# Routed experts on TensorE: 28 steps of two 64-row pieces on two column halves, in place of 31 steps of one 128-row tile

## The reference, cut to what matters

```python
def _moe2_ref(x, w_gate, w_local, w1, w2):
    logits = np.einsum('bsd,de->bse', x, w_gate)
    local_gate = 1.0 / (1.0 + np.exp(-np.einsum('bsd,de->bse', x, w_local).squeeze(-1)))
    for b in range(B):
        prev_e = -1
        for s in range(S):
            fresh_e = int(np.argmax(logits[b, s]))
            if s == 0 or local_gate[b, s] < 0.5:
                e = fresh_e
            else:
                e = prev_e if prev_e >= 0 else fresh_e
            prev_e = e
            ...
            h = np.maximum(x[b, s] @ w1[e], 0.0)
            out[b, s] = p[e] * (h @ w2[e])
```

## Time and profile before

| What | Value |
|---|---|
| Median of 3 runs | 992.57 us (991.91 to 993.82) |
| The profiled execution: its own time | 993.9 us |
| Its span | 992.2 us |
| Granted clock of PE, mean over the span | 0.987 of 2.4 GHz |
| PE busy with matmuls | 947.2 us, 95% of the span |
| DVE, ACT, POOL busy | 465.9, 270.5, 275.8 us |

### The profile page before, as it was taken

The page is one execution under the profiler, slowest core; times in us unless marked ns, Lnnn a source line. Parts: engine busy times, 40 slices in busy tenths (PEclk is TensorE's granted clock), DMA queues, the critical chain, the costliest instruction groups (busy, mean ns, idle before and its releaser), DMA issues.

```text
span 992.2 us, 51897 instructions
## 1 busy us (share of the span) xinstructions
PE 947.2 (95%) x23581; PEld 732.5 (74%) x23582; DVE 465.9 (47%) x964; ACT 270.5 (27%) x503; POOL 275.8 (28%) x297
## 2 busy tenths in 40 slices
PE   4689999999999999999999999999999999999995
PEld 3579989899898996454554554557888888888884
DVE  5447877887887762423143143162352322222220
ACT  1224444444444442201202202202212122122120
POOL 4535566556656651000011010010052101111111
PEclk9789999999999999999999999999999999999999
DMA  5216442333333321780100100047421111001000
GB/s 147 64 50 209 140 123 89 114 104 119 96 115 111 89 72 41 238 271 0 38 27 24 42 28 20 1 133 256 130 88 61 34 34 39 23 28 33 27 29 3
DMA packets 57704, 81.63 MB, mean 82 GB/s; under 512 B 22274, under 2 KB 37454, under 8 KB 57648
## 3 DMA queue, kind: packets, MB, share of 16 engines
q1 hardware_dynamic: 33536, 58.87, 19.0%
q10 hardware_dynamic: 21088, 13.32, 5.2%
q0 software_dynamic: 3024, 8.72, 2.4%
HBM read 68.04 MB, written 14.45 MB: 83 GB/s over the span
## 4 chain that ended last, share of the span: by engine, by line
PE 91%; issue 3%; DVE 2%; DMA 2%; POOL 1%; ACTq 0%; ACT 0%; POOLq 0%; SPq 0%; DVEq 0%
PE ps_D L1478 14%; PE ps_D L224 12%; PE ps_G L1460 6%; PE ps_E L1460 6%; PE ps_B L236 5%; PE ps_E L956 5%; PE ps_B L188 3%; PE ps_G L1467 3%; PE ps_D L1039 3%; PE ps_A L930 3%; PE ps_G L188 3%; PE ps_D L990 2%; PE ps_E L954 2%; PE ps_E L188 2%; PE ps_D L930 2%
## 5 line engine op out<-in xcount | busy, mean ns | idle before, releaser
L1478 PE MATMUL ps_D<-room,hT 128*128 x496 | 139.1, 433 | 0.8 <-issue 0.8
L224 PE MATMUL ps_D<-room 128*128 128x384 f32 x384 | 126.7, 489 | 0.6 <-DVE room L291 0.6
L1478 PEld LDWEIGHTS ps_D<-room,hT 128*128 128x128 f32 x496 | 91.8, 190 | 35.9 <-issue 1.3
L224 PEld LDWEIGHTS ps_D<-room 128*128 128x128 f32 x384 | 72.1, 190 | 51.5 <-issue 1.6
L1421 POOL DMA_INDIRECT out<-y,token x31 | 35.6, 1147 | 258.3 <-DVE y L1585 224.7
L550 POOL DMA_INDIRECT sorted_rows<-rows,slot x24 | 23.9, 997 | 278.3 <-DVE slot L542 272.2
L894 POOL TENSOR_TENSOR room<-room 32x256 f32<-32x256 f32 x96 | 69.5, 724 | 106.5 <-DVE room L1310 101.1
L1521 ACT ACTIVATE hT<-ps_G 128x512 f32<-128x512 f32 x31 | 18.5, 598 | 217.6 <-PE ps_E L1467 211.4
L1585 DVE TENSOR_SCALAR y<-ps_D,x_in 128x320 f32<-128x320 f32 x31 | 17.0, 550 | 125.9 <-PE ps_D L1478 117.5
L1568 DVE COPY w_own<-room 128x1024 f32 x62 | 44.9, 729 | 62.3 <-PE ps_G L1460 33.8
L291 DVE TENSOR_TENSOR room<-ps_D,room 128x384 f32<-128x384 f32 x32 | 17.8, 558 | 113.2 <-PE ps_D L224 107.8
(11 more groups left out here) (225 smaller groups left out, 1646.2 us busy)
## 6 DMA issues: line engine op xcount, KB each, us to landing
room<-in_moe_w SPq DMA_DIRECT2D x8, 1280.0 KB, 12.6
room<-in_moe_w SPq DMA_DIRECT2D x8, 1024.0 KB, 9.2
room<-in_kb SPq DMA_DIRECT2D x48, 160.0 KB
room<-in_vt SPq DMA_DIRECT2D x24, 320.0 KB, 3.1
x_in<-sorted_rows ACTq DMA_DIRECT2D x27, 161.0 KB, 2.3
room<-in_w SPq DMA_DIRECT2D x48, 82.7 KB
room<-in_a SPq DMA_DIRECT2D x48, 80.0 KB
room<-in_r SPq DMA_DIRECT2D x48, 80.0 KB
```

Of the source, the lines that this page charges most:

```text
L224: mm = pe.matmul(self.vs_bank[n % 2][:, 0:TH], self.v[:, s, d * P:(d + 1) * P], self.wspT[:, s, t * TH:(t + 1) * TH], start=(s == 0), stop ...
L1478: mm = pe.matmul(self.ps_y, side.hT[:, u % 2, f, :], self.weights.w2[:, bass.ds(e, 1), f, :], start=(f == 0), stop=(f == self.NF - 1))
```

## The change

A piece is now 64 rows, so that at most 48 + 7 = 55 pieces are needed, and a step takes two pieces, which may belong to different experts: 28 steps (`STEPS`). The two pieces share a step's buffers: rows 0 to 63 and 64 to 127 of `x_in`, of `ps_y` and of the output.

- `hidden`: four quarters instead of two halves: the two pieces times the two halves of the inner features. Each matmul has 64 weight columns and 64 moving columns, and consecutive matmuls alternate between the column halves of the array (outputs at partitions 0 and 64). `w1_own` stays one buffer, so DVE copies each half twice a step (`fetch_w1` with its piece `h`). `w1_rest_own` gets a place for each piece, and the 64-feature part is done for both pieces together behind the four quarters, on four 64x64 tiles.
- `project`: the first piece reads w2 of its expert out of `room`, on the first column half; the second piece reads `w2_own`, a copy that ACT makes once a step (`fetch_w2`), on the second. PE reads its register before `hidden`.
- `fetch`: two table reads and two DMAs of 64 rows.
- The waits of `hidden` and `project` are gathered on a semaphore instruction of its own (`passed`) ahead of the matmuls.
- The tables hold 56 pieces; the first part covers 24 (12 steps) instead of 11 tiles. The operations of the tables have more elements.
- The routing steps of the fourth batch stand at other places (`steps` in `tensor`, `scalar`, `vector`), most of them inside a step, ahead of `project` on PE. `other_tiles` is split in two (`blank_rows` and `other_tiles`), and POOL scatters after 6 puts instead of 3.
- The scratch area for POOL's DMA descriptors is set to 4096 bytes, which makes room for `w2_own`.

```diff
+STEPS = (SORTED_HALVES + 1) // 2
...
-FIRST = (BATCH - 1) * TILES - (EXPERTS - 1)
-NT = 32
+FIRST = 12
+NT = 2 * STEPS
...
     def fetch(self, eng, turn, u):
+        for h in range(2):
+            at = eng.value_load(self.side.tile_at[0:1, bass.ds((turn * self.SLOTS + u) * 2 + h, 1)], min_val=0,
+                                max_val=BLANK_HALF)
+            eng.dma_start(self.side.x_in[h * HALF:(h + 1) * HALF, u, :],
+                          self.by_half[bass.ds(at, 1), :, :].rearrange("o p n -> (o p) n")).then_inc(self.s_in[u], 16)
...
     def hidden(self, pe, turn, u):
...
+        for h in range(2):
+            tokens = slice(h * HALF, (h + 1) * HALF)
+            x = side.xTt[:, u % 2, :, tokens]
+            for half in range(2):
+                pe.wait_ge(self.w1_in, 4 * t + 2 * h + half + 1)
+                if h == 0:
+                    pe.wait_ge(self.h_out, self.FREE + 2 * t + half - 1)
+                pe.sem_inc(self.passed, 1)
+                for f in range(4):
+                    for k in range(NK - 1):
+                        for c in range(2):
+                            lo = (half * 4 + f) * P + c * HALF
+                            mm = pe.matmul(self.ps_h[half][c * HALF:(c + 1) * HALF, f, tokens],
+                                           side.w1_own[:, k, lo:lo + HALF], x[:, k, :],
+                                           start=(h == 0 and f == 0 and k == 0), stop=False, skip_group_check=True)
+                mm.then_inc(self.h_made, 1)
+        pe.wait_ge(self.w1_rest_in, 2 * t + 2)
+        pe.sem_inc(self.passed, 1)
+        for h in range(2):
+            tokens = slice(h * HALF, (h + 1) * HALF)
             for f in range(4):
+                for half in range(2):
+                    kept = slice(half * self.REST, (half + 1) * self.REST)
+                    for c in range(2):
+                        lo = f * P + c * HALF
+                        mm = pe.matmul(self.ps_h[half][c * HALF:(c + 1) * HALF, f, tokens],
+                                       side.w1_rest_own[kept, h, lo:lo + HALF], side.xTt[kept, u % 2, NK - 1, tokens],
+                                       start=False, stop=True, skip_group_check=True)
...
+    def project(self, pe, turn, u, e):
...
+        pe.wait_ge(self.w2_in, t + 1)
...
         for f in range(self.NF):
+            pe.matmul(self.ps_y[first, :], side.hT[:, u % 2, f, first], self.weights.w2[:, bass.ds(e, 1), f, :],
+                      start=(f == 0), stop=(f == self.NF - 1))
+            mm = pe.matmul(self.ps_y[second, :], side.hT[:, u % 2, f, second], side.w2_own[:, f, :],
                            start=(f == 0), stop=(f == self.NF - 1))
...
+    def fetch_w2(self, act, turn, u):
+
+        side, w2, t = self.side, self.weights, turn * self.SLOTS + u
+        e = act.value_load(side.tile_expert[0:1, bass.ds(2 * t + 1, 1)], min_val=0, max_val=self.E - 1)
+        w2.until_loaded(act, e)
+        if not isinstance(turn, int) or t >= 1:
+            act.wait_ge(self.y_made, t)
+        act.activation(side.w2_own[:, :, :], w2.w2[:, bass.ds(e, 1), :, :].rearrange("p o f n -> p (o f) n"),
+                       ACT.Copy).then_inc(self.w2_in, 1)
...
+    def fetch_w1(self, dve, turn, u, h):
...
+            if h == 1:
+                dve.wait_ge(self.h_made, self.part_made(t, 0, half))
+            elif later:
+                dve.wait_ge(self.h_made, self.part_made(t - 1, 1, half))
...
+        steps = {1: routing.turn_rows, 4: routing.turn_back, 5: routing.count}
...
+        steps = {1: turned_rows, 3: lambda: routing.join_rows(act, self.LAST),
+                 4: lambda: routing.copy_expert(act, self.LAST), 5: lambda: routing.copy_counts(act, self.LAST)}
...
+        steps = {0: lambda: routing.choose(dve, self.LAST), 2: lambda: routing.scan(dve, self.LAST),
+                 4: lambda: routing.weigh(dve, self.LAST), 5: lambda: routing.place(dve, self.LAST),
+                 6: lambda: routing.blank_rows(dve), 7: lambda: routing.other_tiles(dve)}
```

More of the change, by code:

```diff
@@ L39 @@
 FIRST_END = 25088
[L40 to L43 removed]
+CAP = TOKENS // HALF
+BLANK_HALF = EXPERTS * CAP
+FIRST = 12
+NT = 2 * STEPS
 PAY = DM + 2
@@ L555, in later @@
         sb = Carver(c.wide, 0, 2 * SEQ)
-        return (sb("over", EXPERTS, CAP), sb("past", NT, EXPERTS), sb("weighed", NT, EXPERTS), sb("te", NT),
-                sb("at", NT), sb("count", EXPERTS), sb("tiles", EXPERTS), sb("upto", EXPERTS), sb("weight", EXPERTS),
+        later = NT - 2 * FIRST
+        return (sb("over", EXPERTS, CAP), sb("past", later, EXPERTS), sb("weighed", later, EXPERTS), sb("te", later),
+                sb("at", later), sb("count", EXPERTS), sb("tiles", EXPERTS), sb("upto", EXPERTS), sb("weight", EXPERTS),
                 sb("need", EXPERTS), sb("blank", PAY))
@@ L627, in other_tiles @@
         dve.tensor_copy(s.blank_slot[:, :], need[:, :]).then_inc(self.blank_slot_d, 1)
+    def other_tiles(self, dve):
+        s, c, link = self.side, self.made, self.link
+        over, past, weighed, te, at, count, tiles, upto, weight, need, blank = self.later(c)
         link(dve, dve.tensor_tensor(weight[:, :], s.first[:, 1:EXPERTS + 1], tiles[:, :], ALU.subtract))
@@ L632, in other_tiles, with fill_blank_half @@
         link(dve, dve.tensor_tensor_scan(upto[:, :], s.ones[:, 0:EXPERTS], tiles[:, :], 0.0, ALU.mult, ALU.add))
-        self.table(dve, c, upto[:, :], weight[:, :], FIRST, SORTED_TILES - FIRST, s.first[:, 0:1], self.all_known)
-    def fill_blank_tile(self, sp):
+        self.table(dve, c, upto[:, :], weight[:, :], 2 * FIRST, NT - 2 * FIRST, s.first[:, 0:1], self.all_known)
+    def fill_blank_half(self, sp):
         blank = self.later(self.made)[-1]
@@ L1414, in sync @@
         weights.load(sp, EXPERTS - 1)
-        routing.fill_blank_tile(sp)
+        routing.fill_blank_half(sp)
     def put(self, pool, turn, u):
@@ L1447, in turn_x, with part_made @@
         mm.then_inc(self.xt_made, 1)
+    def part_made(self, t, h, half):
+        return 5 * t + 2 * h + half + 1
     def hidden(self, pe, turn, u):
         side, t = self.side, turn * self.SLOTS + u
-        x = side.xTt[:, u % 2]
         pe.wait_ge(self.xt_out, self.FREE + t + 1)
-        for half in range(2):
-            pe.wait_ge(self.w1_in, 3 * t + half + 1)
-            pe.wait_ge(self.h_out, self.FREE + 2 * t + half - 1)
-            for f in range(4):
-                col = (half * 4 + f) * P
-                for k in range(NK - 1):
-                    mm = pe.matmul(self.ps_h[half][:, f, :], side.w1_own[:, k, col:col + P], x[:, k, :],
-                                   start=(f == 0 and k == 0), stop=False, skip_group_check=True)
-            mm.then_inc(self.h_made, 1)
@@ L1463, in hidden @@
-        pe.wait_ge(self.w1_in, 3 * t + 3)
-        for f in range(4):
-            for half in range(2):
-                kept = slice(half * self.REST, (half + 1) * self.REST)
-                mm = pe.matmul(self.ps_h[half][:, f, :], side.w1_rest_own[kept, f * P:(f + 1) * P], x[kept, NK - 1, :],
-                               start=False, stop=True, skip_group_check=True)
+        for h in range(2):
[14 more added lines that the diff above has]
+                mm.then_inc(self.h_made, 1)
@@ L1475, in project @@
         pe.wait_ge(self.y_out, self.FREE + t)
         pe.wait_ge(self.h_out, self.FREE + 2 * t + 2)
+        pe.sem_inc(self.passed, 1)
+        first, second = slice(0, HALF), slice(HALF, P)
         for f in range(self.NF):
-            mm = pe.matmul(self.ps_y, side.hT[:, u % 2, f, :], self.weights.w2[:, bass.ds(e, 1), f, :],
+            pe.matmul(self.ps_y[first, :], side.hT[:, u % 2, f, first], self.weights.w2[:, bass.ds(e, 1), f, :],
+                      start=(f == 0), stop=(f == self.NF - 1))
+            mm = pe.matmul(self.ps_y[second, :], side.hT[:, u % 2, f, second], side.w2_own[:, f, :],
@@ L1486, in tile_pe @@
             self.turn_x(pe, *self.at(turn, u, 2))
-        self.project(pe, turn, u)
+        if between:
+            between()
+        self.project(pe, turn, u, e)
     def tensor(self, pe):
@@ L1498, in tensor @@
         self.hidden(pe, 0, 0)
-        routing.turn_rows(pe, self.LAST)
-        self.peeled(pe, self.tile_pe, 0, 2)
-        routing.turn_back(pe, self.LAST)
-        self.peeled(pe, self.tile_pe, 2, 3)
-        routing.count(pe, self.LAST)
-        self.peeled(pe, self.tile_pe, 3, FIRST - 1)
-        pe.wait_ge(routing.all_known, 1)
-        self.peeled(pe, self.tile_pe, FIRST - 1, self.PEELED * self.SLOTS)
+        steps = {1: routing.turn_rows, 4: routing.turn_back, 5: routing.count}
+        for t in range(self.PEELED * self.SLOTS):
+            if t == FIRST - 1:
+                pe.wait_ge(routing.all_known, 1)
+            self.tile_pe(pe, t // self.SLOTS, t % self.SLOTS,
+                         (lambda step=steps[t]: step(pe, self.LAST)) if t in steps else None)
         self.every_tile(pe, self.tile_pe)
```

142 lines of the change are left out of this document (67 added, 75 removed).

## The result

| | median us | runs | ratio to before, 95% |
|---|---|---|---|
| before, on record | 993.09 | 991.91 to 993.82 (4) | |
| the change, on record | 1033.33 | 1031.59 to 1034.57 (4) | 1.0405 [1.0383, 1.0428] |
| the same kernel, control in group 3 | 999.44 | 998.07 to 1000.45 (4) | 1.0083 [1.0066, 1.0100] |
| control in group 4 | 1001.47 | 998.81 to 1007.81 (4) | 1.0101 [1.0045, 1.0156] |
| control in group 5 | 1034.84 | 1034.60 to 1036.08 (3) | 1.0422 [1.0394, 1.0451] |

The change is slower than before in every group of runs, but by 4% in two of them and by 1% in the others, and nothing lies between. Runs of one group are on one chip. The kernel before takes 991.3 to 993.2 in all groups. So there are two questions: where the 33 us come from that only some groups show, and why 8 us over the kernel before remain in the others, which is 12 over the forecast of 987.1.

The account below looks back on a forecast made before the run. PE was taken to bound the kernel, holding nine tenths of the chain that ended last. Terms of -8.5 + 1.6 + 0.9 - 0.8 + 0.8 + 0.5 = -5.5 us gave 987.1 us against the median of 992.57, range 977 to 1001.

Parts of the forecast that it names:

- Column halves overlap: PE's hidden product: matmuls on the two column halves run at once, a quarter taking 1.06 us, four 4.24 against 3.66.
- Rival 1: PE's hidden product and project: in column halves, loads do not overlap matmuls, 55 ns more a round; some 1110 us; 4%.
- The cut of the steps: Experts' part on PE: three of 31 steps go, the others grow from 9.46 to 10.17 us; -8.5 us net.
- 2.06, against two quarters, 2.12. Hidden: DVE's w1 copies: a quarter's weights are ready 2.06 us after the start two quarters before, 0.06 to spare.
- rival 2: DVE's weight copies come onto the path, slower than before: 0.97 us each costs 6.2 us, 1.12 costs 10.4; 21%.
- POOL's scatter and blank rows keep steps of slack.: Routing on POOL: these finish steps before ACT waits for them; no cost was added.
- DVE's last tables get the time under a project, so the 0.82 goes: Routing: PE's 0.82 us wait for weights that DVE copies late, after the routing's tables, disappears; -0.8 us.
- PE's instructions: +0.5.: PE's instruction fetch: 115 matmuls a step in place of 35, fetching just keeps up; +0.5 us (0 to +12).
- x on ACT: +0.9.: Step 1: row-splitting DMAs and small activations on ACT make x late, so PE waits 0.9 us, once.
- The w2 copy in the last step: Before the last project: ACT's w2 copy has no hidden product to cover it, about 2.6 in place of 1.0; +1.6 us.
- The routing steps that I had at nothing beyond -0.8: Routing in the experts' part: only the 0.82 us wait behind DVE's last tables was priced, as a gain of 0.8 us.
- the last project's 0.1: PE's project: a start adds 0.12 us, making the project 4.44 in place of 4.32.

Follow-up runs that it names:

- b1_scratch: The kernel before with only the scratch area for POOL's DMA descriptors set to 4096 bytes: 989.31 us, ratio 0.9981.
- e2_unroll: The changed kernel with PE's loop of four steps written out, other engines keeping theirs: 997.22 us.
- four edits: The changed kernel with, one each, output DMAs held, PE's loop written out, weight loads held, POOL's bursts spread: 1000.41, 997.22, 1000.68, 1001.02 us.

## Why the prediction was wrong

**What held.** Column halves overlap: in the control the quarters follow at 0.93 to 1.16, the four with the 64-feature part take 5.26 (853.15 - 847.89; forecast 5.34), turning 0.48 (0.39), the project 4.36 (4.44), the step 10.10 (10.17). Rival 1, with its 1110, is out: 16 rounds in 0.93 to 1.16 us leave no 55 ns each for a load. The Trainium skill ("TensorE: Matmul & The Clock Gate", Part 3) says that a weight load overlaps a running matmul only where the row group differs, and for the two column halves this trace does not agree. Copies took 0.69 and 2.34 (2.37). The cut of the steps pays where the steps are steady, as forecast.

**The first term that failed on record: "2.06, against two quarters, 2.12. Hidden".** It took DVE's start at 0.15 behind PE's last record, from the step at 828 us of the kernel before. POOL's put lay across that step too, and the copy began on time in it, 0.45 into the put:

```profile
827.93 1.26 POOL L1421 DMA_INDIRECT out<-y,token  x1 [8.19 <-DVE y L1585]
```

So one row beside a put was taken for all. On record, beside a put, the start was 1.05 behind, and with 0.06 to spare the fourth quarter began up to 0.7 us late, 18 times: 11.2 us. This is rival 2 by its place, copies on the path, and nearly by its size (6.2 to 10.4), but not by its mechanism: it priced copies that last longer, and the copies kept their 0.69; it is their start that was late.

**The larger one: "POOL's scatter and blank rows keep steps of slack."** True for those who wait for the rows. I did not price the bursts for those who work beside them: 20.9 us on record, with 8.0 of "issue" in the 64-feature part and 11.8 of longer matmul records. The trace of before had carried 14 such DMAs beside 35 matmuls a step at 0.82 us of PE's time, and I read that wait as the price of the routing's tables. The rows in the group of b1_scratch above show three starts, on ACT and DVE, 1.8 to 2.1 us late ahead of it, and without them there is no wait. So the term "DVE's last tables get the time under a project, so the 0.82 goes" had the wrong cause.

**"PE's instructions: +0.5."** The mechanism was named, its size was wrong, in every condition. The rate in steady steps is kept up with. The loss is at two kinds of place that the rate does not tell. At the start, beside the weight loads: 5.6 us (22.76 against 17.13). At the loop's two jumps, 2.0 us each in this control (in others the steps there are up to 4 us longer than their neighbours); the row of the first, in the control, and the rows over 1 us of what PE waited for in 800 to 996 us when the loop is written out (e2_unroll):

```profile
870.15 1.15 PE L1478 MATMUL ps_G<-xTt,w_own 128*64 128x64 f32 x32 [1.96 <-issue]
```

```profile
PE ps_D L1509 <- ACT w_own L1565: 3.1, 1, 3.1
PE ps_G L1478 <- DVE w_own L1617: 1.4, 3, 0.6
```

No "issue" before L1478 is left, and the kernel is 2 to 4 us shorter. The Trainium skill ("Runtime: NRT & Kernel Launch", Instruction fetch mechanics) says that a taken branch whose target isn't held stalls on its fetch, and these rows agree. It calls the cost of crossing a block "mostly hidden"; if the 3.3 us of "issue" beside full DMA engines are such a crossing, which no run shows, this one was not.

**"x on ACT: +0.9."** 2.57, and in the control 1.6 more through the granted clock, after PE had stood. The DMA issues took 2.06 where I had 1.57 for the pair, and the two half fetches 1.80 where I had 0.35 + 0.35 + a read of 0.72. **The w2 copy in the last step**, +1.6: the wait was 3.1 in place of 2.6. Behind it the control of group 4 has a granted clock of 0.74 and takes 9.32 us between its last two evictions, where the one of group 3 has 1.00 and 7.63; the forecast had no term for that. The routing steps that I had at nothing beyond -0.8 added 2.1 in steps 4 and 5 (11.94 and 10.49 us in the control).

The sum for the control, from the first hidden product to the last project (985.97 - 685.56 = 300.4; before 978.42 - 686.34 = 292.1): the forecast for that stretch was 292.1 - 8.5 + 1.6 + 0.9 - 0.8 + 0.5 less the last project's 0.1, 285.7. Above it: start 6.6 (5.6 through the loads, 1.0 beyond), x 3.2, jumps 4, routing 2.1, last step 0.5, less 0.07 in each of some 22 steps, 1.5: 14.9 for the 14.7, or 14.4 without the 0.5 that the forecast had for instructions. The controls, 999.4 and 1001.5, lie at the end of the range (977 to 1001) and half a us beyond it, and on the wrong side of 993; on record another 33 us lie outside every case I had.

## What to carry to other kernels

When a change multiplies an engine's instructions, price the places where its stream is cut off (a loop's jump, the start of a new part, full DMA engines) apart from its rate; and put reads into registers where a long instruction covers them. A wait of before that the change is to remove needs its cause looked up first: the 0.82 us here had another. When a handshake has less than a microsecond of slack, look for what other engines do at that moment, POOL's indirect DMAs above all, and place those under the longest instructions of the step; that cost nothing where it was not needed. Rerun the unchanged kernel before any edit of it is read: four edits "cured" what most likely was not there in their group.

## What was not expected of the hardware

- The same program on the same kind of chip takes 999 to 1001 us in some groups of runs and 1033 to 1035 in others, all runs of a group alike, while the kernel before moves by 0.2%. What sets the condition was not found. The record gives the groups of 999.4 (group 3) and of 1034.8 (group 5) the same chip number; if that is one chip, the chip alone does not set it.
- In the condition of the record DVE starts 1.05 us behind the last record of a quarter that ends about 0.4 us into an indirect DMA of POOL (1.15 to 1.24 us long), 0.15 otherwise, and PE stands in "issue" between its 64x64 matmuls while POOL issues six or eight indirect DMAs: 18.6 and 22.7 us a step in place of 10.1 and 10.3, with a granted clock of 0.82 and 0.77.
- A put takes 0.98 us alone and 1.34 to 1.36 with a DVE copy of w1 that starts 0.5 into it.
- A read into a PE register between two matmul groups is hidden with 35 matmuls a step and costs 0.4 us of each step with 115.
